# Scores of the second batch in two matmul passes instead of three, with high queries and low queries sharing one stationary tile

## The reference

```python
scores = scale * q @ k.T                       # per head; 768 x 768, depth 64
scores = where(is_sink | in_window, scores, -1e9)
a = exp(scores - max); a = a / (sum(a) + 1e-09)
x = a @ v                                      # heads side by side: (2, 768, 512)
u = x + (xt @ U @ V).T;       x = u + relu(u @ w_ch1) @ w_ch2          # mixer 1
u = x + (relu(xt @ t1) @ t2).T; out = u + relu(u @ w1) @ w2            # mixer 2
```

## Time and profile before

| | |
|---|---|
| median of 3 runs | 653.14 us (652.93 to 653.2) |
| profiled execution | 653.0 us |
| its span, first to last instruction | 651.2 us |
| PE busy | 630.7 us, 97% |
| DVE, ACT, POOL busy | 331.8, 317.2, 367.0 us |
| granted TensorE clock | full in every slice |

### The profile page before, as it was taken

The page is one execution under the profiler, slowest core; times in us unless marked ns, Lnnn a source line. Parts: engine busy times, 40 slices in busy tenths (PEclk is TensorE's granted clock), DMA queues, the critical chain, the costliest instruction groups (busy, mean ns, idle before and its releaser), DMA issues.

```text
span 651.2 us, 10345 instructions
## 1 busy us (share of the span) xinstructions
PE 630.7 (97%) x3532; PEld 565.3 (87%) x3532; DVE 331.8 (51%) x721; ACT 317.2 (49%) x719; POOL 367.0 (56%) x373
## 2 busy tenths in 40 slices
PE   6999999999999999999999999999999999999997
PEld 5888798899889897899999988889998888899986
DVE  7776542333343344377567662186668325676411
ACT  4657555454454453565445444454444455444321
POOL 8545456656555565356756554475756543757262
PEclk9999999999999999999999999999999999999999
DMA  8344254342322515223232333233233342421142
GB/s 180 91 92 118 46 162 115 98 130 81 98 82 82 161 51 161 58 72 112 67 113 82 109 98 102 82 113 99 80 113 98 95 139 91 146 87 44 49 134 93
DMA packets 88276, 65.51 MB, mean 101 GB/s; under 512 B 43008, under 2 KB 72192, under 8 KB 88224
## 3 DMA queue, kind: packets, MB, share of 16 engines
q1 hardware_dynamic: 88224, 64.85, 34.8%
HBM read 61.42 MB, written 3.15 MB: 99 GB/s over the span
## 4 chain that ended last, share of the span: by engine, by line
PE 87%; DVE 4%; ACT 3%; issue 3%; POOL 2%; DMA 0%; ACTq 0%; DVEq 0%; POOLq 0%
PE bank L1356 33%; PE bank L1155 21%; PE bank L1322 10%; PE bank L1185 4%; PE bank L1212 4%; PE bank L1193 3%; PE bank L1286 3%; PE bank L1249 3%; PE bank L1230 2%; PE bank L1170 1%; PE bank L1263 1%; POOL w_lo L753 1%; ACT w_hi L774 1%; PE bank L1348 1%; DVE x_nat L978 1%
## 5 line engine op out<-in xcount | busy, mean ns | idle before, releaser
L753 POOL TENSOR_TENSOR w_lo<-w_raw,w_hi 128x512 fp32r<-128x512 f32 (+1 forms) x158 | 205.6, 1307 | 170.9 <-ACT w_hi L774 170.4
L774 ACT ACTIVATE w_hi<-w_raw 128x512 fp32r<-128x512 f32 (+1 forms) x158 | 96.4, 618 | 60.6 <-PE bank L1356 42.7
L1155 PE MATMUL bank<-b_hi,a_hi 128*128 128x384 f32 x280 | 94.8, 338 | 1.0 <-DVE temps L1065 0.6
L1155 PE MATMUL bank<-b_lo,a_hi 128*128 128x384 f32 x280 | 94.8, 339 | 0.0
L1356 PE MATMUL bank<-w_hi,hid_hi 128*128 128x512 f32 x216 | 87.6, 406 | 0.0
L1356 PE MATMUL bank<-w_hi,hid_lo 128*128 128x512 f32 x216 | 85.1, 394 | 0.0
L1356 PE MATMUL bank<-w_lo,hid_hi 128*128 128x512 f32 x216 | 84.7, 392 | 0.0
L800 ACT ACTIVATE probs<-masked,neg_max 128x264 f32<-128x264 f32 x96 | 49.5, 516 | 68.3 <-DVE neg_max L953 67.8
L1356 PE MATMUL bank<-w_hi,y_hid 128*128 128x512 f32 x216 | 71.1, 394 | 0.2
L953 DVE CUSTOM_DVE_ANT_0 masked<-bank,masks 128x264 f32<-128x264 f32 x96 | 41.2, 430 | 39.5 <-PE bank L1185 35.6
L898 DVE SCALAR_TENSOR_TENSOR hid_lo<-bank,hid_hi 128x384 fp32r<-128x384 f32 x32 | 17.8, 558 | 77.6 <-ACT hid_hi L762 77.6
(11 more groups left out here) (137 smaller groups left out, 1405.8 us busy)
## 6 DMA issues: line engine op xcount, KB each, us to landing
w_raw<-in_moe_w_ch_dram SPq DMA_DIRECT2D x144, 256.0 KB, 2.7
w_raw<-in_moe_w_ch_dram SPq DMA_DIRECT2D x20, 512.0 KB, 3.4
q_nat<-in_q_dram SPq DMA_DIRECT2D x12, 256.0 KB, 3.0
k_nat<-in_k_dram SPq DMA_DIRECT2D x12, 256.0 KB, 3.5
v_nat<-in_v_dram SPq DMA_DIRECT2D x12, 256.0 KB, 3.3
out_dram<-o_stage SPq DMA_DIRECT2D x12, 256.0 KB, 3.4
w_raw<-in_moe_w_tok_dram SPq DMA_DIRECT2D x6, 256.0 KB, 2.7
w_raw<-in_moe_w_tok_dram SPq DMA_DIRECT2D x8, 192.0 KB, 2.3
```

The costliest lines, as they stand in the source:

```text
L753: nc.gpsimd.tensor_tensor(w_lo[:, split % NW, 0:n], w_raw[:, split % NR, 0:n], w_hi[:, split % NW, 0:n].bitcast(f32), ALU.subtract) \
L774: nc.scalar.activation(w_hi[:, split % NW, 0:n], w_raw[:, split % NR, 0:n], ACT.Copy) \
L1155: last = mm(bank[:, 0:HALF], w[at % 2][:, a, k, :], u[:, b_part, k, :], start=(first and n == 0), stop=(n == 5), skip_group_check=True)
```

## The change

It concerns tiles 6 to 11. A new tile `q_both` has, for each pair of heads, two planes. In plane e (0 even, 1 odd) the rows of head e hold the low queries and the rows of the other head hold the high queries of head e. The keys `k_hi` hold, in plane e, the high keys of head e on both halves of the rows instead of zeros on one. One pass of `q_both` by `k_hi` then gives low by high and high by high together, and with `q_hi` by `k_lo` a unit has two passes.

To fill the other half, DVE makes two more casts of 64 rows right behind the cast of `q_hi`, each from one half of the rows to the other; POOL makes the low queries in two instructions of 64 rows instead of one of 128, the second waiting for the first; and in step `ksplit` ACT copies the keys of each head to the other half (two copies of 64x512; for tile 6 also two of the sink keys, 64x48). PE waits for the new semaphores `q_moved` and `k_moved` ahead of a tile's first scores. DVE signals `q_high`, for which POOL waits, behind the first of its three casts. The tile `above_probs` goes and `a_hi_odd` takes its place in the layout.

```diff
             q_hi = eb("q_hi", [P, 2, PAIRS, P], f32r)
-            q_lo = eb("q_lo", [P, 2, PAIRS, P], f32r)
+            q_both = eb("q_both", [P, 2, PAIRS, 2, P], f32r)
+            q_lo = q_both[:, :, :, 0, :]
...
+        def queries_split(T):
+
+            return T + 1 if T < NQ else 2 * (T + 1) - NQ
+
-        def query_low(eng, T):
+        def query_low(eng, wait, T):
 
+            if T >= NQ:
+                for e in range(2):
+                    rows = slice(e * D, (e + 1) * D)
+                    wait(q_split, queries_split(T - 1) + e)
+                    eng.tensor_tensor(q_both[rows, T % 2, :, e, :], q_full[rows],
+                                      q_hi[rows, T % 2, :, :].bitcast(f32), ALU.subtract).then_inc(q_split, 1)
+                wait(q_split, queries_split(T))
+                return
...
                 elif s[0] == "qsplit" and s[1]:
                     pool.wait_ge(q_high, s[1] + 1)
-                    query_low(nc.gpsimd, s[1])
+                    pool.wait_ge(psink_ready, copied)
+                    if split:
+                        pool.wait_ge(wlo_ready, split)
+                    query_low(nc.gpsimd, pool.wait_ge, s[1])
...
+                elif s[0] == "ksplit" and s[1] >= NQ:
+                    T = s[1]
+                    act.wait_ge(k_copied, T + 1)
+                    act.wait_ge(scores_ready, H * T if T == NQ else H * (T - 1))
+                    for e in range(2):
+                        there = slice((1 - e) * D, (2 - e) * D)
+                        src, _, sinks, _ = list(key_parts(k_hi, T))[e]
+                        if T == NQ:
+                            nc.scalar.activation(k_hi[there, :, e, :, P:BLK], sinks, ACT.Copy)
+                        last = nc.scalar.activation(k_hi[there, :, e, T % 3, 0:P], src, ACT.Copy)
+                    last.then_inc(k_moved, 1)
...
                     nc.vector.tensor_copy(q_hi[:, T % 2, :, :], q_full).then_inc(q_high, 1)
+                    if T >= NQ:
+                        for e in range(2):
+                            rows, there = slice(e * D, (e + 1) * D), slice((1 - e) * D, (2 - e) * D)
+                            moved = nc.vector.tensor_copy(q_both[there, T % 2, :, e, :], q_full[rows])
+                        moved.then_inc(q_moved, 1)
...
-                    for n, (qs, ks) in enumerate(((q_hi, k_hi), (q_hi, k_lo), (q_lo, k_hi))):
-                        last = mm(bank[:, 0:NK], qs[:, T % 2, h // 2, :], keys(ks, T, h // 2, h % 2),
-                                  start=(n == 0), stop=(n == 2))
+                    high, low = q_hi[:, T % 2, h // 2, :], q_lo[:, T % 2, h // 2, :]
+                    if T < NQ:
+                        passes = ((high, k_hi), (high, k_lo), (low, k_hi))
+                    else:
+                        passes = ((q_both[:, T % 2, h // 2, h % 2, :], k_hi), (high, k_lo))
+                    for n, (queries, ks) in enumerate(passes):
+                        last = mm(bank[:, 0:NK], queries, keys(ks, T, h // 2, h % 2),
+                                  start=(n == 0), stop=(n == len(passes) - 1))
```

More of the change, by code:

```diff
@@ L350, in attention_then_two_mixers @@
         temps = sb("temps", [P, 3, HALF])
-        sb("above_probs", [P, 32])
+        a_hi_odd = sb("a_hi_odd", [P, 7, 2, P], f32r)
         w1_sums = sb("w1_sums", [P, 3, 2, P])
         w1_raw = sb("w1_raw", [P, 2, KD, 2 * P])
-        a_hi = [sb(f"a_hi{i}", [P, 7, 2, P], f32r) for i in range(2)]
+        a_hi = [sb("a_hi_even", [P, 7, 2, P], f32r), a_hi_odd]
         a_lo = [sb("a_lo_even", [P, 7, 2, P], f32r), a_lo_odd]
@@ L403, in attention_then_two_mixers @@
         q_high = sem("q_high")
+        q_moved = sem("q_moved")
+        k_moved = sem("k_moved")
         q_split = sem("q_split")
@@ L726, in _ @@
                     pool.wait_ge(psink_ready, copied)
-                    pool.wait_ge(q_split, s[1] + 1)
+                    pool.wait_ge(q_split, queries_split(s[1]))
                     if split:
@@ L779, in _ @@
                     if T:
-                        act.wait_ge(q_split, T)
+                        act.wait_ge(q_split, queries_split(T - 1))
+                    if T > NQ:
+                        act.wait_ge(q_moved, T - NQ)
                     act.wait_ge(tp_ready, tp_at[s] + 1)
@@ L787, in _ @@
                         act.wait_ge(k_split, keys_split(T - 1))
+                    if T > NQ:
+                        act.wait_ge(k_moved, T - NQ)
                     act.wait_ge(tp_ready, tp_at[s] + 1)
@@ L921, in _ @@
                     nc.vector.tensor_copy(q_hi[:, T % 2, :, :], q_full).then_inc(q_high, 1)
+                    if T >= NQ:
[3 more added lines that the diff above has]
+                        moved.then_inc(q_moved, 1)
                     if T == 0:
                         dve.wait_ge(q_high, 1)
-                        query_low(nc.vector, T)
+                        query_low(nc.vector, dve.wait_ge, T)
                 elif s[0] == "ksplit":
@@ L1176, in _ @@
                     if h == 0:
-                        pe.wait_ge(q_split, T + 1)
+                        pe.wait_ge(q_split, queries_split(T))
+                        if T >= NQ:
+                            pe.wait_ge(q_moved, T - NQ + 1)
+                            pe.wait_ge(k_moved, T - NQ + 1)
                         pe.wait_ge(k_split, keys_split(T) - (2 if T % NQ == 0 else 1))
```

## The result

The changed kernel takes 655.38 us (median of 6 runs, 654.41 to 655.53), the kernel before 653.1 us (6 runs, 652.93 to 653.2). The ratio is 1.0029, with an interval of 1.0019 to 1.004: slower by 0.3%. The forecast was 654.8 us. The profiled execution took 655.48 us, with a span of 653.7 against 651.2 us.

What follows compares the result with a forecast made beforehand. PE was taken as the bound, working 87% of the span. From 653.0 us profiled, -3.5 for passes, +4.9 for casts and +0.3 for ACT's copies gave 654.7, or 654.8 as median; range 650.4 to 656.6.

Steps and rivals of the forecast that it cites:

- 48 passes fewer: PE in batch 1: 48 units lose a pass, 29 of them give 0.12 us each, 3.5 us saved.
- casts, tiles 7, 8, 9, 10, 11: DVE's two added casts delay the masking in the `qsplit` units, so PE waits: 4.9 us in all.
- casts, tile 6: Inside batch 0's attention the mask comes 0.2 us later, behind cover of more than a unit: costs nothing.
- ACT's copies of tile 6: ACT's key copies delay the last `probs_T` at the end of batch 0: 0.3 us, range 0.1 to 0.6.
- POOL's second half: One more POOL instruction of about 1.28 us per tile, covered by over 4 us before `w_lo` is used: nothing.
- casts together: Rival, `qsplit` units: DVE does both casts back to back, POOL after; costs 1.1 us, time 650.7 us, chance 0.19.
- turns: Forecast case, `qsplit` units: DVE and POOL alternate whole instructions, second cast ending 1.86 us behind `q_hi`; 4.9 us, chance 0.56.
- lower bound: Casts run back to back, masking 0.86 us later: 0.66 us at tile 7, 0.07 at tiles 8 and 9, 0.8 in all.
- Partly covered: Rival: PE is ahead after the saved passes, so half the cast stalls go; 652.4 us, chance 0.13.
- POOL first: Rival, `qsplit` units: POOL goes ahead of the first cast and again ahead of the second; 657.5 us, chance 0.08.

Runs made afterwards that it cites:

- passes alone: The kernel before with the third pass (low queries by high keys) left out in the second batch and nothing added: 650.31 us, ratio 0.9952.
- POOL last: The changed kernel with POOL's query-split halves, from tile 6 on, waiting until both of DVE's copies into `q_both` are done: 650.92 us, ratio 0.9968.
- additions alone: The changed kernel with all its additions but three passes in the second batch, high queries by low keys done twice: 658.34 us, ratio 1.0072.
- key copies later: The changed kernel with ACT's four key copies for tile 6 moved behind the first batch's last probability copies: 654.23 us, ratio 1.0014.

## Why the prediction was right

The time (655.4 against 654.8; 654.5 in the two runs at the full clock) and the side were right. The mechanism was the one forecast, but part of the closeness is luck: two terms that it lacked nearly cancel, the lower clock (+1.1) and the layout (-1.15).

| step | forecast | measured |
|---|---|---|
| 48 passes fewer | -3.5 | -3.2 by unit 95 and at the full clock (passes alone), -2.9 in the medians |
| casts, tiles 7, 8, 9, 10, 11 | 1.8, 1.25, 1.25, 0, 0.6 | 1.90, 1.22, 1.24, 0, 0.56 |
| casts, tile 6 | 0 | +0.12, at unit 46 |
| ACT's copies of tile 6 | +0.3 | +0.1 to +0.3 |
| POOL's second half | 0 | 0, no wait for `w_lo` |
| POOL's new wait in batch 0 | not priced | about +0.2, within the scatter of the start |
| granted clock, 75 to 80 us | not priced | about +1.1 where it falls |
| layout of the stationary tiles | not priced | -1.15 |

- What a pass is worth: 0.12 us, as read from the earlier trace rows, where PE goes straight on. 29 units were to give it, 27 did, and unit 94 gave some back. The passes that turned into waits did so where the earlier trace rows had shown the bank to be the limit.
- The casts: the choice between casts together (1.1 us in all) and turns (4.9 us) decided the sign. The small POOL copy that got in between two casts pointed the right way, but it was thin evidence: the second of those casts still took 0.42 us, so that row shows POOL not waiting, and not a DVE cast that waits. The 1.14 and 0.29 us that follow come from the other pair of rows, and these held. POOL last shows the cause, since with POOL held back the same casts are done in 0.86 us. That it came out at 650.9 us, near the 650.7 of the rival in which the casts stay together, is partly chance: that rival lacked the 1.15 us of the layout and had the bare casts 0.6 us too cheap.
- The bare casts cost 1.4 us instead of the 0.8 of the lower bound: tiles 8 and 9 lose 0.22 and 0.25 us where 0.07 was worked out, and tile 7 0.92 where 0.66 was.
- Tile 6: the mask behind its casts comes 0.26 us later in the trace (0.2 forecast), but the cover doesn't hold all of it, and unit 46 starts 0.12 us late in every kernel that has them. POOL's second half for tile 6 stands in the same kernels and isn't told apart from them.
- Partly covered: refuted by additions alone. POOL first: its sign, a first cast of over 1 us, isn't there; the first cast took 0.42 us at each tile.
- "ACT's copies": mechanism and size right. The step that they make in the trace is larger because the clock fell in the same place.
- Missing were three lines of the change that looked like bookkeeping: the spacer that went, and the two waits ahead of POOL's query split, which also hold in batch 0.

## What to carry to other kernels

Before you put DVE work behind an instruction for which POOL waits, look at what POOL will start at that moment: here two casts cost 4.9 us ahead of the masking, 1.4 us with POOL held back, and some 0.3 us two units later. A saved matmul is worth its start-to-start distance only in units where PE doesn't then wait for something that began ahead of it; count those units (27 of 48 here). And read the allocations in a diff as part of it: a spacer of 128 bytes moved this kernel by about 1 us.

## What the runs showed of the hardware that was not expected

- Place of a stationary tile: 840 matmuls of 384 columns start 0.1760 us apart in the layout of the kernel before, and 0.1745 in four layouts with three of the four stationary tiles moved by 128, 384 or 448 bytes from there, up to whole steps of 512.
- Between two DVE casts of 64x512 that follow each other at once, a POOL subtraction that has been waiting gets in: 1.83 to 1.85 us for the pair at tiles 7, 8, 9 and 11, the same in additions alone and key copies later, and 0.86 with POOL held back. The masking, whose input is in PSUM, takes 0.43 us with POOL's half running beside it and 0.43 without.
- The granted clock can fall at the same place (75 to 80 us, 0.66 instead of 1.00) in a kernel whose instructions are those of the kernel before and only the allocations differ.
